# An attention recurrence with one scan over four head pairs and its constants in SBUF, instead of two half scans with constants in PSUM

## What is computed

```
for t in range(S):
    cur = u * k_t (outer) v_t
    y[t] = r_t @ (state + cur)
    state = w_t[:, None] * state + k_t (outer) v_t
```

## Time and profile before

| | us |
|---|---|
| median of 3 runs | 789.22 |
| lowest and highest | 786.07 and 792.0 |
| the profiled execution, its own time | 788.66 |
| its span, first to last instruction | 786.9 |

### The profile page before, as it was taken

How to read it: one execution, slowest core, us unless ns; L and a number is a source line. 1 busy time by engine, 2 the same in 40 slices (tenths; PEclk the granted TensorE clock), 3 DMA queues, 4 the chain that set the end, 5 groups by cost and what they waited for, 6 DMA issues and landing times.

```text
span 786.9 us, 20291 instructions
## 1 busy us (share of the span) xinstructions
PE 725.5 (92%) x5566; PEld 645.7 (82%) x5567; DVE 498.7 (63%) x1359; ACT 389.9 (50%) x761; POOL 161.8 (21%) x202
## 2 busy tenths in 40 slices
PE   2898898884899999999999999799999999999994
PEld 2687787773799999999999998699999999999993
DVE  7899999996567584747586584464444445336521
ACT  3656776873446453636455563154443535235421
POOL 5454665664000000000000000000111000000000
PEclk9999999996999999999999999999999999999997
DMA  6555589643843360513363352363433333315110
GB/s 134 152 143 145 162 249 255 174 129 116 280 153 128 112 195 26 168 63 124 109 200 105 114 168 73 113 192 107 142 108 122 122 127 113 120 35 196 40 35 27
DMA packets 50268, 103.75 MB, mean 132 GB/s; under 512 B 7921, under 2 KB 29904, under 8 KB 50224
## 3 DMA queue, kind: packets, MB, share of 16 engines
q1 hardware_dynamic: 29536, 67.18, 27.4%
q10 hardware_dynamic: 15568, 21.76, 10.4%
q0 software_dynamic: 5120, 14.26, 4.9%
HBM read 85.73 MB, written 19.01 MB: 133 GB/s over the span
## 4 chain that ended last, share of the span: by engine, by line
PE 75%; DVE 9%; issue 5%; DMA 4%; ACT 2%; SPq 1%; POOL 1%; ACTq 1%; POOLq 0%; DVEq 0%
PE bank L1372 19%; PE bank L1398 19%; PE bank L1406 10%; PE bank L1377 9%; PE bank L1387 6%; PE bank L1361 2%; PE bank L1339 2%; DMA rk<-rk_in 2%; DVE SF L797 2%; DVE Q L788 2%; PE bank L1188 1%; PE bank L1332 1%; ACTq L524 1%; PE bank L1275 1%; PE bank L1253 1%
## 5 line engine op out<-in xcount | busy, mean ns | idle before, releaser
L1372 PE MATMUL bank<-wall,xT_hi 128*128 (+1 forms) x660 | 177.6, 404 | 1.3 <-ACT xT_hi L678 1.3
L1398 PE MATMUL bank<-wall,hT_hi 128*128 x880 | 164.8, 338 | 0.5 <-ACT hT_hi L687 0.5
L1398 PEld LDWEIGHTS bank<-wall,hT_hi 128*128 128x128 f32 x880 | 153.0, 188 | 3.3 <-issue 0.9
L1372 PEld LDWEIGHTS bank<-wall,xT_hi 128*128 128x128 f32 x660 | 117.6, 189 | 21.4 <-issue 1.8
L912 DVE TENSOR_TENSOR wall<-raw,wall 128x1024 f32 (+1 forms) x96 | 112.0, 1221 | 28.0 <-ACT wall L579 28.0
L682 ACT ACTIVATE hs<-bank 128x512 f32<-128x512 f32 x110 | 65.3, 593 | 126.6 <-PE bank L1377 126.6
L579 ACT ACTIVATE wall<-raw 128x1024 f32 (+1 forms) x96 | 95.2, 1051 | 10.7 <-issue 9.6
L1087 DVE TENSOR_TENSOR xT_lo<-bank,xT_hi 128x384 fp32r<-128x384 f32 x57 | 31.8, 558 | 106.8 <-ACT xT_hi L678 106.8
L687 ACT ACTIVATE hT_hi<-bank 128x512 fp32r<-128x512 f32 x110 | 59.8, 596 | 69.9 <-PE bank L1387 67.7
L1377 PE MATMUL bank<-wall,xT_lo 128*128 (+1 forms) x330 | 93.9, 393 | 0.0
L1406 PE MATMUL bank<-wall,hT_lo 128*128 x440 | 91.2, 349 | 0.0
(11 more groups left out here) (206 smaller groups left out, 989.1 us busy)
## 6 DMA issues: line engine op xcount, KB each, us to landing
raw<-wall_in SPq DMA_DIRECT2D x96, 512.0 KB, 5.1
xin<-sorted ACTq DMA_DIRECT2D x59, 194.0 KB, 2.5
rk<-rk_in SPq DMA_DIRECT2D x46, 192.0 KB
v_in<-v_src ACTq DMA_DIRECT2D x24, 192.0 KB, 3.5
vT<-vT_in ACTq DMA_DIRECT2D x48, 96.0 KB, 4.2
wb<-w_in SPq DMA_DIRECT2D x46, 96.0 KB
sorted<-padrow SPq DMA_DIRECT2D x16, 194.0 KB, 2.3
out<-ybuf,toki POOLq DMA_INDIRECT x28, 2.6
```

What stands on the lines that cost most here:

```text
L1372: pe.matmul(bank[n][:, :], xT_hi[:, k, :], w[:, bass.ds(slot, 1), cols].rearrange("p o n -> p (o n)"), start=(k == 0 and w is w_hi), stop= ...
L1398: pe.matmul(bank[2][:, 0:DM], hT_hi[:, j, :], w[:, bass.ds(slot, 1), W2 + j * DM:W2 + (j + 1) * DM].rearrange("p o n -> p (o n)"), start=( ...
```

## The change

Both scans of a unit cover all four pairs in one instruction (516 and 515 elements instead of twice 258 and twice 257), and their rows of constants, first_q and last_q, are tiles of their own in SBUF. The reciprocals of all four pairs are one instruction. The wait for SF moves from in front of Rq to in front of Kb. The start clears three rows in place of two. The semaphore counts follow.

```diff
             SF = sb1("SF", [P, SEG])
+            first_q = sb1("first_q", [P, SEG])
+            last_q = sb1("last_q", [P, SEG - 1])
...
-            link(v.memset(bank[7][:, :], 0.0))
-            link(v.memset(bank[7][:, 0:HSEG:C1], 1.0))
+            link(v.memset(first_q[:, :], 0.0))
+            link(v.memset(first_q[:, 0::C1], 1.0))
+            link(v.memset(last_q[:, :], 0.0))
...
-                for hf in range(2):
-                    v.tensor_tensor_scan(Q[:, kq, hf * HSEG:(hf + 1) * HSEG], wb[:, par, hf * HSEG:(hf + 1) * HSEG], bank[7][:, 0:HSEG],
-                                         1.0, ALU.mult, ALU.add).then_inc(q_ready, 1)
-                v.wait_ge(q_ready, 2 * u + 2)
+                v.tensor_tensor_scan(Q[:, kq, :], wb[:, par, 0:SEG], first_q[:, :], 1.0, ALU.mult, ALU.add).then_inc(q_ready, 1)
+                v.wait_ge(q_ready, u + 1)
 
                 whole = Q[:, kq].rearrange("p (a t) -> p a t", t=C1)
-                for hf in range(2):
-                    v.reciprocal(bank[7][:, LASTQ + C - 1:LASTQ + HSEG - 1:C1], whole[:, 2 * hf:2 * hf + 2, C]).then_inc(iq_ready, 1)
-                    v.wait_ge(iq_ready, 2 * u + hf + 1)
-                    top = (hf + 1) * HSEG - 2
-                    v.tensor_tensor_scan(SF[:, top:(None if hf == 0 else HSEG - 1):-1], wb[:, par, top + 2:hf * HSEG + 1:-1],
-                                         bank[7][:, LASTQ + HSEG - 2:LASTQ - 1:-1], 1.0, ALU.mult, ALU.add).then_inc(sf_ready, 1)
-                    v.wait_ge(sf_ready, 2 * u + hf + 1)
+                v.reciprocal(last_q[:, C - 1::C1], whole[:, :, C]).then_inc(iq_ready, 1)
+                v.wait_ge(iq_ready, u + 1)
+                v.tensor_tensor_scan(SF[:, SEG - 2::-1], wb[:, par, SEG:1:-1], last_q[:, ::-1], 1.0, ALU.mult, ALU.add).then_inc(sf_ready, 1)
                 route()
                 v.tensor_tensor(Rq[:, k], rk[:, par, 0], whole[:, :, 0:C], ALU.mult).then_inc(r_ready, 1)
+                v.wait_ge(sf_ready, u + 1)
                 v.tensor_tensor(Kb[:, k], rk[:, par, 1], SF.rearrange("p (a t) -> p a t", t=C1)[:, :, 0:C], ALU.mult).then_inc(k_ready, 1)
```

More of the change, by code:

```diff
@@ L33 @@
 SEG = PAIRS * C1
-HSEG = SEG // 2
-LASTQ = C1 + 2
 JC = F // P
```

## The result

The changed kernel took 793.32 us (median of 14 runs, 790.92 to 798.23), the kernel before 788.94 in the same comparison (14 runs, 785.41 to 793.38). The ratio is **1.0058**, with an interval of 1.0040 to 1.0077: 4.6 us slower (0.58% of 789; the two medians themselves lie 4.4 us apart), less than a single run can tell. The span of the profiled execution grew from 786.9 to 791.3 us. The forecast was 795.

A forecast was written before the change was run, and what follows sets the result against it. DVE's chain in the attention was taken as the bound. Terms -14.4 + 10.4 + 14.7 - 4.3 - 0.6 = +5.8 us on the profiled 788.66 make 794.5; as that run lies 0.56 below the median, 795 us, range 780 to 805.

The forecast's parts named there:

- the likeliest case: The forecast itself for the whole changed kernel: 795 us, with its own range of 790 to 801; chance 0.45.
- What bounds the kernel: In the attention, DVE's chain sets the time: busy 26.6 to 27.1 us of 27.7 to 28.8 per four units.
- The scans, -14.4 us: Merging both DVE scans and the reciprocals saves 0.60 us in each of 24 units, 14.4 us in all.
- (a): POOL's decay meets DVE's Q scan in 20 units and gets the ports; the scan waits 0.52 us: +10.4 us.
- the lower end: If the Q scan gets the ports, 0.29 us of the decay sticks out behind it: 5.8 us.
- (b): POOL's two masks take turns with DVE between Q scan and Kb: 0.78 us in 17 units, +14.7 us together.
- (c): What masks already cost Kb and Rq today, 4.3 us, is contained in the masks' term and taken off.
- Waits, -0.6 us: DVE's wait of 0.61 us for a load goes, since loads keep their place and DVE comes later.
- Rival A: DVE's scans don't take part in the turns with POOL: 9.6 us less, 779.6 us; chance 0.17.
- Rival B: POOL's scatter takes turns too, so SF waits 0.7 us at 14 scatters: +9.8 us, 804.8 us; chance 0.20.
- Rival C: Only the decay costs; masks find room elsewhere or wait without harm: -4.6 us, 784.6 us; chance 0.18.

The follow-up runs named there:

- halves in SBUF: Kernel before with only its row of constants moved to SBUF, scans and reciprocals still in two halves: 801.20 us, ratio 1.0141.
- Q alone: Kernel before with only Q's scan merged and its constants in SBUF, SF still in halves with constants in PSUM: 793.21 us, ratio 1.0045.
- the gated kernel: Changed kernel in which POOL, in units with a scatter, waits for DVE's next Kb before making the masks: 795.15 us, ratio 1.0072.

## Why the prediction was right, point by point

The kernel became slower by the mechanism named, turns between scans and POOL's masks, and the time fell into the likeliest case's own range. That it fell within 2 us of 795 is luck in part: one term was far too large, and another too small by less.

*What bounds the kernel*: held. DVE is busy 29.12 of 29.84 us in four units. Of the first units up to the Q scan in the last one, DVE's busy time rose by 7.7 us (0.5 + 7.2) and its idle time fell by 6.1; together the 1.6 us by which that scan comes later.

*The scans, -14.4 us*: mechanism right, size nearly. (The listing of DVE's order before has six waits, not the five that the text under it counts.) The Q scan is 1.22 us (1.19 forecast), SF 1.23 (1.21). From the reciprocal to Rq it is 110.86 - 109.49 = 1.37 us in the unit shown (1.33 forecast, 1.86 before). From the Q scan's start to the reciprocal it is 1.24 us, 0.06 less than before, and with the 0.49 behind it 0.55 us a unit, 13.2 in all. An access to SBUF that is cheaper by 65 ns did not show: the reciprocal of 2 elements has 168 ns with its output in SBUF (halves in SBUF) against 175 in PSUM, and the shortest Q scan of 258 elements 664 against 657. The Trainium skill's figures for that ("Perfetto Trace Analysis", section "Optimizing Scalar/DVE Operations") have no support in these traces.

*(a) The decay, +10.4 us*: **the step that failed.** "I take the first", the decay gets the ports, was wrong. It is the Q scan that gets them and the decay that waits, 1.45 to 1.54 us in place of 0.52 in 19 of its 20 units. Nor did the lower end's 0.29 us come: the decay ends 0.30 us behind the scan, and the SF scan, due 0.24 behind it, keeps its 1.23 us. What the Q scans lose beyond their median is (1354 - 1219) x 24 = 3.2 us, most of it in two that met not the decay but a mask with rkp behind it. One of these:

```profile
76.07 1.22 POOL L406 TENSOR_SCALAR_AFFINE_SELECT AT<-AT 128x512 f32<-128x512 f32 x2
76.99 2.63 DVE L788 TENSOR_TENSOR_SCAN Q<-wb,first_q 128x516 f32<-128x516 f32 x1
77.26 1.26 POOL L398 TENSOR_TENSOR rkp<-rk 128x512 f32<-128x512 f32 x1
```

The decay's loss comes back through POOL's order: with the decay, and in three of five cases the scatter, made late by the scans, the masks land on Kb. Q alone, where only the decay is late, has Kb at 793 ns.

*(b) The masks, +14.7 us*: right in kind and near in size, by places that were partly others. Kb has (1090 - 684) x 23 = 9.3 us, Rq (795 - 680) x 23 = 2.6, SF (1245 - 1230) x 24 = 0.4. The step "in the 4 units with gates1 the second falls beside operations with one input" was wrong: a TENSOR_SCALAR of one input waits like the others (L879, 611 ns for 170), and so did one CAST of four. The five groups of the routing shown above have 1.7 us more for each four units, 6.9 in all, with those of two inputs. Kb loses more than the 0.44 us I took, where two masks go ahead of it in one piece. So (a) and (b) are about 22.4 us, against 25.1 forecast: the sum was right because an overrated decay covered underrated masks. The pair without masks puts a second number beside it: masks cost 13.8 us now and nothing that can be told before.

*(c) Today's cost, -4.3 us*: by the groups it stands, but taking the masks out of the kernel before gave nothing that can be told at the marker. DVE then waited longer for PE and loads (3.0 and 2.9 us for 1.2 and 2.1). So a part of the 4.3 us had hidden other waits, and the term was too large; by how much is open.

*Waits, -0.6 us*: underrated. In the kernel before, DVE waited 3.8 us for loads and their issue and 1.2 us for PE up to the last unit; after, 1.0 us for a load and none for PE. 4 us of waits are gone, since DVE itself is later.

With these, the sum reads -13.2 + 22.4 - 4.3 - 4.0 = +0.9 us where the Q scan of the last unit has +1.6 and the marker +2.0 in the first trace of before, +4.2 in the second. The times themselves say +4.6 (0.0040 to 0.0077 of 789, or 3.2 to 6.1 us).

*Rival A* (scans take no part) falls with the constants moved alone: halves of 808 and 851 ns. *Rival B* (the scatter takes turns) is half right: it waits, 1.83 us for 1.01, but Kb beside it stays at 0.68. (The 1.04 ns an element in its price is 1.02 by its own terms, which changes nothing.) *Rival C* (masks find room) falls with the 13.8 us; its value for a kernel without mask costs, -4.6 us, was itself too small beside the measured -10.7, since it priced the decay at 10.4 where all that the Q scans lose is 1.0.

Two things are not shown. The first is what decides whether POOL or DVE gets the ports; it is not settled by who has waited longer. In a unit without scatter they alternate, the second mask between Rq and Kb:

```profile
40.21 1.23 DVE L794 TENSOR_TENSOR_SCAN SF<-wb,last_q 128x515 f32<-128x515 f32 x1
40.23 2.68 POOL L406 TENSOR_SCALAR_AFFINE_SELECT AT<-AT 128x512 f32<-128x512 f32 x2
41.36 1.06 DVE L796 TENSOR_TENSOR Rq<-rk,Q 128x512 f32<-128x512 f32 x1
42.34 1.11 DVE L798 TENSOR_TENSOR Kb<-rk,SF 128x512 f32<-128x512 f32 x1
```

while behind a scatter both masks pass ahead of Kb in one piece, and Kb was kept out from 111.44 although their recorded start is 111.78. A mask that is queued behind a running scatter seems to hold DVE out before it starts in the record; the gated kernel agrees (no mask queued, no hold), and so do the small operations: L852 and L879 take 0.70 us beside a scatter with masks behind it in the changed kernel. Beside a scatter with none behind it the first takes 0.16 us in the gated kernel, and the second 0.17 in the changed kernel without masks. The scan of 1.96 us above, due while rkp was on with the decay next, fits too. None of them shows more. The second is what merged scans with constants in PSUM would give, the gain of merging without the turns. They were not tried: the two rows of constants need 516 + 515 columns where the bank that DVE has to itself holds 512.

## What to carry to other kernels

Before an operand of a long DVE instruction is moved from PSUM to SBUF, look at what GpSimd does beside it; the operand in PSUM may be what keeps the two engines apart, and here it was worth 11 us. Follow the engine that loses a meeting to its next instructions: the decay's wait cost nothing where it stood, and together with the scatter's it set where the masks fell. Where a change has parts, time each: SF's merging alone was 0.35% faster and Q's alone 0.45% slower, and the two together were a small loss.

## What the runs showed of the hardware

Some operations with one input take part in the turns too. DVE and POOL in the routing of the changed kernel:

```profile
86.79 1.83 POOL L420 DMA_INDIRECT sorted<-rows,slot  x1 [0.16 <-issue]
87.91 0.70 DVE L852 TENSOR_TENSOR r<-r,ssq 128x4 f32<-128x4 f32 x1
88.64 1.23 POOL L406 TENSOR_SCALAR_AFFINE_SELECT AT<-AT 128x512 f32<-128x512 f32 x2
88.64 0.67 DVE L853 TENSOR_TENSOR r<-r 128x4 f32<-128x4 f32 x1
89.34 0.55 DVE L854 TENSOR_SCALAR r<-r 128x4 f32<-128x4 f32 x1
```

and a CAST beside the masks of the next unit (rows between them left out):

```profile
97.67 1.23 POOL L406 TENSOR_SCALAR_AFFINE_SELECT AT<-AT 128x512 f32<-128x512 f32 x2
98.28 0.65 DVE L901 CAST oh<-placed 128x8 bf16<-128x8 f32 x1
```

L852 waits beside the scatter, with the masks behind it, and L853 beside the masks. A TENSOR_SCALAR of 4 elements takes 0.55 us beside the masks (0.17 before), and the one CAST of L901's four that starts beside a mask 0.65 (the others 0.16 to 0.17), while beside the same masks a RECIPROCAL (L880) keeps its 0.18 us and a TENSOR_REDUCE of 32 elements (L894) its 0.18. An indirect DMA's instruction on POOL waits for a scan of two SBUF inputs (1.83 us for 1.01) without holding DVE in turn, as far as the gated kernel shows. And the mean granted clock of TensorE is 0.98 in both stretches before, and 1.00 and then 0.95 after, in the stretch with scatters. There it lies at half for 3.4 us from 93.0, 123.7 and 161.3 us, the lower of its two levels (1.2 GHz). PE was busy 84.08 us of that stretch of 95.68. In this trace the clock cost the attention nothing up to there, since DVE did not wait for PE once.
